# Order of the first product's units in the attention steps, and of VectorE's work where the second layer begins

## The chip, the cores and the metric

One NeuronCore of a Trainium2 chip runs the whole program: TensorE (matmuls), VectorE, ScalarE, GpSimd and SyncE (SP, which issues the loads and stores), each with its own list of instructions, bound to each other by semaphores alone. The metric is the device time of one execution in microseconds (us), from repeated runs. Beside it there is one profiled execution, whose trace gives the start and length of every instruction.

## The reference

Attention with a soft cap over 2 x 12 heads of 448 positions and 64 columns, then two feed-forward layers on the 896 tokens of width 768, with an inner width of 2048:

```python
scores = cap * tanh((q @ k.T / sqrt(64)) / cap)
attn = exp(scores - max(scores)); attn /= sum(attn) + 1e-9
x = (attn @ v) as (896, 768)
x = elu(x @ w_in) @ w_out            # first layer
x = leaky(x @ w_in2, 0.01) @ w_out2  # second layer
```

## The kernel before, in words

**Numbers in two parts.** Each f32 operand of TensorE is kept as a rounded high part (`..._hi`) and the low rest (`..._lo`), and a **product** of one 128 x 128 weight block with 448 columns is three matmuls: high x high, high weight x low data, low weight x high data (`product`, lines 1127 to 1131). The high part is made by ScalarE, the low part by a subtraction on VectorE or GpSimd, after the high part.

**Attention steps.** The attention of 24 heads is cut into 48 half heads (slots). One step `s` of 55 has, on TensorE in this order (lines 1220 to 1240): the 8 transposes of slot s-2, products of the first layer placed "before scores", the four score matmuls of slot s+1, products "before values", in odd steps 8 matmuls of values, and products "after values". ScalarE does tanh(s), the exponentials of slot s-1, `hidden(u)` for each unit that ended in step s-1, the high part of the probabilities of slot s-2, and the weight copy `w_high(u + 3)` for each such unit (lines 698 to 707). VectorE does the maxima, the end of `hidden(u)`, the low part of the probabilities (line 765) and, in turn, the reciprocals and the scaling of the outputs. From slot 23 on the transposes of a step wait for the low part of the slot before (lines 1094 to 1098). GpSimd's list has, per step (from line 568): the low part of the weights `split_w(u + 3)` of each unit that ended in the step before, in odd steps the split of v, every fourth step (the last is step 53) `x_parts(m)`, three instructions that make two parts of the attention's output, and in even steps the split of k and q.

**Units.** The first product of layer 1 (x @ w_in) is done in units, two batches of 16. Unit u is 128 of the 2048 columns; it takes KC = 6 products (u, c), c = 0 to 5, that add up in one of three PSUM banks. Product c needs the output of heads 2c and 2c+1. A unit **ends** with c = 5. Its end releases `hidden(u)` (two ScalarE instructions and one on VectorE, which free its bank), ScalarE's copy of the weights of unit u+3, GpSimd's split of the same weights (line 559), and SP's load of raw weights of unit u+7. A product waits for the split of its unit's weights. Where the products of the first batch stand is written by hand: `EARLY` (steps 24 to 30), `MIXED` (how many at each of the three places of a step) and `LATER` (in which order). Behind step 54 the 16 units of the second batch run one after the other.

**Second products, blocks.** The other three big products of the two layers use a 7-product form of the 2 x 2 block product (p1 to p7). p5, p6, p3 and p7 need sums of weight blocks (`weight_sum`, VectorE, line 880) and sums of data (`x_sum`, line 899). After the second product of layer 1 (`second(0)`), the first product of layer 2 runs in blocks i = 0 to 7 of seven, in the order `BLOCK_SEQ`: (0, p3), (0, p7), (0, p1), (0, p5), (0, p6), (1, p1), (1, p5), (1, p6), (1, p3), (1, p7), (0, p2), (0, p4), (1, p2), (1, p4), and then (2, p1) and so on; they are called items 0, 1, 2, ... Each is 3 products, 9 matmuls, into one PSUM bank; the eight banks go round, so (1, p3) takes the bank of (0, p3), and waits until `block_hidden(0, "p3")` has read it.

**The border** is the stretch in which layer 2's data are made. On VectorE `x_low(p)` (line 895) is the low part of the data of p, after ScalarE's `x_high(p)` (line 652). The data of p5, p6 and p4 are the second, third and fourth data sum. `add_to(0, "p4", ...)` (line 891) finishes the last quarter of layer 1's result. `block_add(i, p)` (lines 944 to 957) gathers the blocks' sums, ScalarE's `leak(i, p)` (line 672) scales one by 0.01, `block_hidden(i, p)` (line 962) takes the maximum and frees the bank. `block_keep(i)` (line 664) is ScalarE's copy of p1's bank, and `block_add(i, "p6")` waits for it.

ScalarE's list at the border is fixed: weight copies of items 0 and 1, `x_high("p1")`, items 2 and 3, `x_high("p5")`, items 4 and 5, `x_high("p6")`, items 6, 7, 8 and 9, `block_keep(0)`, `x_high("p2")`, items 10 and 11, `leak(0, "p3")`, item 12, `leak(0, "p7")`, item 13, `x_high("p4")`, `block_keep(1)`. A weight copy of an item with a sum waits for that sum: items 8 and 9 are (1, p3) and (1, p7). GpSimd's list is the splits of the same items.

Of the kernel before, what the change touches and what calls it, by code (L numbers as in the profile page):

```python
# [1 line left out]

# [7 lines left out]
ALU = mybir.AluOpType  # L10
# [10 lines left out]
KC = D_MODEL // P  # L21
# [3 lines left out]
MAT_UNITS = FC  # L25
# [19 lines left out]

TWO_BANKS = 10
EARLY = {24: ((0, (0, 1, 2)),), 25: ((0, (3,)),), 26: ((1, (0, 1, 2)),), 27: ((1, (3,)),), 28: ((2, (0, 1, 2)),),
         29: ((2, (3,)),), 30: ((0, (4,)), (1, (4,)), (2, (4,)))}

FIRST_LOADS = (7, 11, 15, 19, 23, 26, 29)  # L50
STEPS = 55
# [2 lines left out]

MIXED = {31: (0, 0, 1), 32: (0, 1, 0), 33: (0, 2, 0), **{s: (2, 2, 0) for s in range(34, 48, 2)},
         **{s: (1, 1, 0) for s in range(35, 48, 2)}, 48: (2, 1, 0), 49: (1, 2, 0), 50: (2, 1, 0), 51: (2, 0, 4),
         52: (0, 0, 6), 53: (0, 0, 6), 54: (0, 0, 8)}


def early_chunks(u):  # L60
# [1 line left out]

LATER = [(0, 5), (1, 5), (3, 0), (3, 1), (2, 5)] + [(u, c) for u in range(3, MAT_UNITS) for c in range(KC) if u > 3 or c > 1]


def chunks_at(s):

    if s in EARLY:  # L70
        return [], [], EARLY[s]
    done = sum(sum(n) for t, n in MIXED.items() if t < s)
    places = []
    for n in MIXED.get(s, (0, 0, 0)):
        place = {}
        for u, c in LATER[done:done + n]:
            place.setdefault(u, []).append(c)
        places.append(list(place.items()))
        done += n
    return places  # L80

# [84 lines left out]
def build(nc, qT, kT, v, w, cap, out, inv_rows):  # L166
    with ExitStack() as ctx:
# [584 lines left out]
        def _(dve):  # L752
# [89 lines left out]
            def weight_sum(n):  # L842
                stage, p, j = item_name(n)
                raws = ITEM_RAWS[n]
                for r in raws:
                    dve.wait_ge(*loaded(r))
                if stage == "blocks":
                    dst, (lo, hi) = w_source(n), (slice(0, HALF), slice(HALF, UNIT))
                    if j >= 2:
                        dve.wait_ge(*split_done(GEMM1 + BLOCK_AT[j - 2, p]))  # L850
                    else:
                        dve.wait_ge(*split_done(GEMM1 - 9))
                    if p == "p6" or p == "p3":
                        ahead = GEMM1 + BLOCK_AT[j, SUMS[SUMS.index(p) - 1]]
                        dve.wait_ge(*sum_done(ahead))
                        before = w_source(ahead)
                    a11, a12 = w_raw[:, raws[0] % RAW, lo], w_raw[:, raws[0] % RAW, hi]
                    if p == "p5":
                        args = a11, a12, ALU.add
                    elif p == "p7":  # L860
                        args = a11, w_raw[:, raws[1] % RAW, lo], ALU.subtract
                    elif p == "p6":
                        args = before, a11, ALU.subtract
                    else:
                        args = a12, before, ALU.subtract
                else:
                    dst, one = s_sum[:, j, :], w_raw[:, raws[0] % RAW, :]
                    if p == "p5":
                        if stage == "second1":
                            dve.wait_ge(*split_done(GEMM2[1] - 3))  # L870
                        args = one, w_raw[:, raws[1] % RAW, :], ALU.add
                    else:
                        dve.wait_ge(*split_done(n - PQ))
                        if p == "p7":
                            args = one, w_raw[:, raws[1] % RAW, :], ALU.subtract
                        elif p == "p6":
                            args = dst, one, ALU.subtract
                        else:
                            args = one, dst, ALU.subtract
                nc.vector.tensor_tensor(dst, *args).then_inc(s_done, 1)  # L880
# [6 lines left out]
            def add_to(l, p, dst, kept, there):  # L887

                dve.wait_ge(pair_done, product_end(l, p))
                for t in range(HC):  # L890
                    nc.vector.tensor_tensor(dst[:, t, :], kept[:, t, :], banks_of[l][p][t], ALU.add).then_inc(there, 1)

            def x_low(p):
                dve.wait_ge(xc_hi_done, X_GROUPS.index(p) + 1)
                nc.vector.tensor_tensor(x_parts_of[p][1][:, :, :], x_source[p][:, :, :], f32(x_parts_of[p][0][:, :, :]),
                                        ALU.subtract).then_inc(xc_split, 1)

            def x_sum(dst, a, b, op):
                nc.vector.tensor_tensor(dst[:, :, :], a[:, :, :], b[:, :, :], op).then_inc(x_sum_done, 1)
# [38 lines left out]
            def block_add(i, p):  # L938

                ps, u2, p1 = block_bank(i, p), block_u2[i % 2], block_p1[i % 2]  # L940
                dve.wait_ge(unit_done, product_no(i, p))
                if p == "p6":
                    dve.wait_ge(block_p1_kept, i + 1)
                    nc.vector.tensor_tensor(u2, p1, ps, ALU.add).then_inc(block_u2_done, 1)
                    dve.wait_ge(block_u2_done, i + 1)
                    nc.vector.tensor_tensor(block_u4, u2, block_bank(i, "p5"), ALU.add).then_inc(block_u4_done, 1)
                if p == "p3":
                    dve.wait_ge(block_u4_done, i + 1)
                    nc.vector.tensor_tensor(ps, block_u4, ps, ALU.add).then_inc(h_done, 1)
                if p == "p7":  # L950
                    nc.vector.tensor_tensor(u2, u2, ps, ALU.add).then_inc(block_u3_done, 1)
                    dve.wait_ge(block_u3_done, i + 1)
                    nc.vector.tensor_tensor(ps, block_u4, ps, ALU.add).then_inc(h_done, 1)
                if p == "p2":
                    nc.vector.tensor_tensor(ps, p1, ps, ALU.add).then_inc(h_done, 1)
                if p == "p4":
                    nc.vector.tensor_tensor(ps, u2, ps, ALU.add).then_inc(h_done, 1)

            def block_hidden(i, p):
                dst = {"p3": b12, "p7": b22, "p2": b11, "p4": b21}[p]  # L960
                dve.wait_ge(leak_done, quarter_no(i, p))
                nc.vector.tensor_tensor(dst[:, i, :], act_g[:, quarter_no(i, p) % 2, :], block_bank(i, p), ALU.max
                                        ).then_inc(quarter_done, 1)
# [51 lines left out]
            x_low("p1")  # L1015
            dve.wait_ge(xc_split, X_GROUPS.index("p1") + 1)
            x_sum(y12, y12, y11, ALU.subtract)
            weight_sum(GEMM1 + BLOCK_AT[1, "p3"])
            x_low("p5")
            x_sum(y11, y22, y11, ALU.add)  # L1020
            weight_sum(GEMM1 + BLOCK_AT[1, "p7"])
            x_low("p6")
            dve.wait_ge(u3_done, HC)
            add_to(0, "p4", y21, kept_u2[0], y21_done)
            for q in range(GEMM1 + 1, GEMM2[1] + 1):

                i, p = BLOCK_SEQ[q - GEMM1 - 1]
                if i == 0 and p == "p6":
                    x_low("p2")
                if p == "p6":  # L1030
                    block_add(i, "p6")
                if i == 0 and p == "p6":
                    block_add(0, "p3")
                    block_add(0, "p7")
                    block_hidden(0, "p3")
                    block_hidden(0, "p7")
                    dve.wait_ge(xc_split, X_GROUPS.index("p2") + 1)
                    x_sum(y21, y21, y11, ALU.subtract)
                if i == 1 and p == "p5":
                    x_low("p4")  # L1040
                if i and p in ("p3", "p7") or p in ("p2", "p4"):
                    block_add(i, p)
                    k = quarter_no(i, p) - 2
                    if p != "p3":
                        block_hidden(*RESULTS[k])
                if i >= 2 and p == "p1":
                    block_hidden(i - 1, "p4")

                if i == 3 and p in ("p1", "p5", "p3"):
                    c = ("p1", "p5", "p3").index(p)  # L1050
                    first_difference(1, c)
                    third_difference(1, c)
                if i >= 3 and p == "p4":
                    first_difference(1, i)
                    third_difference(1, i)
                if q + 8 < GEMM2[1] and q + 8 >= GEMM1 + 14 and q + 8 in SUM_ITEMS:
                    weight_sum(q + 8)
                if q in (GEMM2[1] - 4, GEMM2[1] - 2):
                    g_low(1, (q - GEMM2[1] + 4) // 2)
# [223 lines left out]
```

## Time and profile before

| | |
|---|---|
| median of 3 runs | 575.11 us (574.1 to 576.91) |
| profiled execution | 574.71 us, span of its trace 572.9 us |
| instructions | 8610 |
| attention steps | step 30 starts on TensorE at 99.12, step 54 at 195.23 |
| second product of layer 1 ends, blocks begin | 360.60 |
| last stall at the border ends | 383.05 |

How to read it: times in the trace are us from the start of the span. PE is TensorE, DVE VectorE, ACT ScalarE, POOL GpSimd. Matmuls overlap, so the time of one is read from start to start, not from its length. A bracket at a row's end tells how long the engine stood idle before it, and which instruction's end released it. "x4" means that four alike were merged into one row. The chain and the waits name the instruction that came last.

### The profile page before, as it was taken

Reading aid. Unit: us, or ns where it says so; the run is one execution under the profiler, and the core shown is the slowest. Engines: PE = TensorE matmul, PEld = TensorE weight load, DVE = VectorE, ACT = ScalarE, POOL = GpSimd, SP = SyncE. Lnnn points to the kernel's source line nnn. Section 1 sums busy time; section 2 is a strip of 40 time slices with the busy share of each in tenths; the row PEclk is TensorE's granted clock in tenths of the full one; section 3 lists DMA queues with packets and bytes.
Section 4 is the critical chain, followed back from the end, with each engine's and each line's share of the span. In section 5 each row is a group of like instructions: output and inputs, shape, how many; then the busy total and the mean of one; then the engine's idle time right before and its main releaser. Section 6 shows DMA issues by size and latency. Waiting matters only on the chain.

```text
span 572.9 us, 8610 instructions
## 1 busy us (share of the span) xinstructions
PE 556.7 (97%) x2908; PEld 499.4 (87%) x2908; DVE 469.4 (82%) x758; ACT 352.8 (62%) x606; POOL 275.2 (48%) x273
## 2 busy tenths in 40 slices
PE   6999989999999999999999999989999999999997
PEld 5777779889998999999999999879999998999997
DVE  5899998878875133898988999889999779999881
ACT  6999988999995455654644454536454445544440
POOL 6779998799965655552000003856666530000000
DMA  6455564455423333335644332031113225536251
GB/s 174 106 143 128 150 174 125 123 130 146 98 65 89 98 112 110 111 108 165 213 135 158 131 99 67 1 110 56 57 55 90 77 84 192 159 119 220 84 170 51
DMA packets 34172, 67.07 MB, mean 117 GB/s; under 512 B 6864, under 2 KB 18768, under 8 KB 34128
## 3 DMA queue, kind: packets, MB, share of 16 engines
q1 hardware_dynamic: 33984, 66.28, 39.4%
q8 instruction: 24, 0.39, 0.3%
q14 instruction: 20, 0.16, 0.1%
q10 hardware_dynamic: 144, 0.23, 0.1%
HBM read 63.70 MB, written 2.80 MB: 116 GB/s over the span
## 4 chain that ended last, share of the span: by engine, by line
PE 77%; DVE 10%; ACT 4%; issue 3%; POOL 3%; DMA 2%; ACTq 0%; SPq 0%; DVEq 0%; POOLq 0%
PE mlp_ps L1129 8%; PE mlp_ps L1131 8%; PE mlp_ps L1130 8%; PE o_ps L1129 6%; PE o_ps L1131 6%; PE o_ps L1130 6%; PE scores L1129 4%; PE scores L1130 4%; PE scores L1131 4%; PE probs_t L1103 4%; PE probs_t L1131 4%; PE probs_t L1130 4%; PE probs_t L1129 4%; PE scores L1088 2%; PE o_ps L1122 2%
## 5 line engine op out<-in xcount | busy, mean ns | idle before, releaser
L559 POOL TENSOR_TENSOR w_lo<-w_raw,w_hi 128x768 fp32r<-128x768 f32 (+1 forms) x62 | 104.2, 1681 | 62.3 <-ACT w_hi L621 61.9
L559 POOL TENSOR_TENSOR w_lo<-s_sum,w_hi 128x384 fp32r<-128x384 f32 x32 | 38.8, 1228 | 114.5 <-ACT w_hi L621 114.5
L621 ACT ACTIVATE w_hi<-s_sum 128x768 fp32r<-128x768 f32 (+1 forms) x64 | 43.4, 684 | 76.6 <-DVE s_sum L880 51.9
L621 ACT ACTIVATE w_hi<-w_raw 128x768 fp32r<-128x768 f32 (+1 forms) x77 | 56.5, 737 | 31.1 <-PE o_ps L1131 15.7
L601 ACT ACTIVATE soft<-soft,neg_max 112x448 f32<-112x448 f32 x96 | 63.6, 673 | 1.8 <-DVE soft L758 1.7
L758 DVE TENSOR_SCALAR_CACHE_REDUCE soft<-soft,neg_abs 112x448 f32<-112x448 f32 x96 | 60.9, 671 | 2.2 <-ACT soft L591 1.9
L1129 PE MATMUL mlp_ps<-x_hi,w_hi 128*128 128x448 f32 x132 | 49.2, 373 | 0.4 <-issue 0.4
L765 DVE TENSOR_TENSOR p_lo<-probs_t,p_hi 112x896 fp32r<-112x896 f32 x37 | 40.3, 1089 | 10.0 <-ACT p_hi L610 9.9
L1130 PE MATMUL mlp_ps<-x_lo,w_hi 128*128 128x448 f32 x132 | 48.2, 365 | 0.0
L1131 PE MATMUL mlp_ps<-x_hi,w_lo 128*128 128x448 f32 x132 | 48.2, 365 | 0.0
L591 ACT ACTIVATE soft<-scores 112x896 f32<-112x896 f32 x47 | 43.4, 924 | 6.0 <-PE scores L1089 5.9
L1088 PE MATMUL scores<-k_hi,q_stack 128*112 128x448 f32 x94 | 36.7, 390 | 4.6 <-ACT soft L591 2.8
L1103 PEld LDWEIGHTS probs_t<-ident,soft 112*112 112x112 f32 x296 | 30.5, 133 | 8.5 <-issue 4.1
L1103 PE MATMUL probs_t<-ident,soft 112*112 112x112 f32 x296 | 34.6, 260 | 3.0 <-DVE p_lo L765 2.3
L610 ACT ACTIVATE p_hi<-probs_t 112x896 fp32r<-112x896 f32 x37 | 33.9, 916 | 5.5 <-PE probs_t L1103 5.5
L803 DVE SCALAR_TENSOR_TENSOR b<-act_g,mlp_ps 128x448 f32<-128x448 f32 x22 | 13.6, 619 | 28.6 <-ACT act_g L630 28.5
L1089 PE MATMUL scores<-k_lo,q_stack 128*112 128x448 f32 x94 | 34.3, 365 | 0.0
L880 DVE TENSOR_TENSOR s_sum<-w_raw 128x768 f32<-128x768 f32 (+1 forms) x32 | 29.4, 920 | 3.8 <-DMA w_raw<-w_units 2.1
L884 DVE TENSOR_TENSOR w_lo<-s_sum,w_hi 128x768 fp32r<-128x768 f32 x32 | 30.4, 950 | 1.5 <-ACT w_hi L621 1.5
L839 DVE TENSOR_TENSOR g_first<-b,g_first 128x896 fp32r<-128x896 f32 x24 | 29.9, 1247 | 0.8 <-ACT g_first L640 0.8
L839 DVE TENSOR_TENSOR g_last<-b,g_last 128x896 fp32r<-128x896 f32 x24 | 27.8, 1160 | 2.2 <-ACT g_last L640 2.2
L628 ACT ACTIVATE act_g<-mlp_ps 128x448 f32<-128x448 f32 x22 | 11.9, 540 | 24.9 <-PE mlp_ps L1131 24.9
(238 smaller groups left out, 1747.7 us busy)
## 6 DMA issues: line engine op xcount, KB each, us to landing
w_raw<-w_units SPq DMA_DIRECT2D x120, 384.0 KB, 3.2
q_raw<-qT SPq DMA_DIRECT2D x24, 224.0 KB, 3.1
k_raw<-kT SPq DMA_DIRECT2D x23, 224.0 KB, 3.0
v_raw<-v_rows SPq DMA_DIRECT2D x24, 112.0 KB, 3.2
inv_all<-inv_rows SPq DMA_DIRECT2D x24, 112.0 KB, 3.4
y_t<-y_out SPq DMA_DIRECT2D x12, 224.0 KB, 2.8
inv_rows<-row_inv SPq DMA_DIRECT2D x24, 1.8 KB, 3.1
k_raw<-kT ACTq DMA_DIRECT2D x1, 224.0 KB, 3.1
```

The source lines that it names most:

```text
L559: pool.tensor_tensor(w_part(w_lo, n), w_source(n), f32(w_part(w_hi, n)), ALU.subtract).then_inc(w_lo_pool, 1)
L591: nc.scalar.activation(soft[0:QT, k % SOFT, :, :], scores_of(k)[0:QT, :, 0:SEQ], ACT.Tanh, scale=scale_reg).then_inc(tanh_done, 1)
L601: nc.scalar.activation(soft[0:QT, b, t, :], soft[0:QT, b, t, :], ACT.Exp, bias=neg_max[:, c, t:t + 1], scale=-1.0, accum_out=row_sum[:, h ...
L621: nc.scalar.activation(w_part(w_hi, n), w_source(n), ACT.Copy).then_inc(w_hi_done, 1)
L758: nc.vector.tensor_scalar(soft[0:QT, b, t, :], soft[0:QT, b, t, :], neg_abs[0:QT, 0:1], BIG, ALU.mult, ALU.min, accum_out=neg_max[:, c, t: ...
L765: nc.vector.tensor_tensor(p_lo[:, h % 2, :, cols].rearrange("p (a b) q -> p a b q", a=2), probs_of(k)[0:QT, :, 0:SEQ].rearrange("p a (b q) ...
L839: nc.vector.tensor_tensor(parts[:, 2:4, :], g_source(l, n)[0], f32(parts[:, 0:2, :]), ALU.subtract).then_inc(g_split, 1)
L1088: nc.tensor.matmul(dst[0:QT, t, 0:SEQ], q_stack[:, b, rows], k_hi[:, b, :], start=True, stop=False)
L1103: last = nc.tensor.transpose(probs_of(k)[0:QT, c // 2, col:col + 2 * QT - 1:2], soft[0:QT, k % SOFT, t, c * QT:(c + 1) * QT], ident[:, :])
L1129: nc.tensor.matmul(dst, w_hi[:, r, blk], hi, start=start, stop=False)
L1130: nc.tensor.matmul(dst, w_hi[:, r, blk], lo, start=False, stop=False)
L1131: return nc.tensor.matmul(dst, w_lo[:, r, blk], hi, start=False, stop=stop)
```

## The change

Three things change, and nothing is added or taken away in what is computed.

First, the order of the first batch's products. Before, a unit's last product (c = 5) came ahead of the first product of the next unit but one, and units 0 to 3 ended in steps 31, 32, 34 and 35. Now c = 4 and 5 of a unit come among the first products of the next: unit u ends in step 2u + 31 up to unit 9 (31, 33, 35, ... 49), units 10, 11 and 12 in steps 51, 52 and 53, and 13, 14 and 15 in step 54 (before: unit 3 in 35, 4 in 37, ... 10 in 49, 11 in 51, 12 in 52, 13 in 53, 14 and 15 in 54). Step 30 has one product in place of three, step 54 ten in place of eight. Step 54 is now (14, 3), (13, 5), (14, 4), (15, 0 to 3), (14, 5), (15, 4), (15, 5). `chunks_at` groups only neighbours of the same unit, so that this order is kept.

Second, on VectorE, ahead of the blocks: the third data sum directly behind the second; `weight_sum` of (1, p7) behind the three adds of p4.

Third, on VectorE, in block 0: `x_low("p2")` behind the adds of p6 and p3 instead of ahead of them, and `block_hidden(0, "p3")` ahead of `block_add(0, "p7")`.

```diff
-         29: ((2, (3,)),), 30: ((0, (4,)), (1, (4,)), (2, (4,)))}
+         29: ((2, (3,)),), 30: ((0, (4,)),)}
...
-         52: (0, 0, 6), 53: (0, 0, 6), 54: (0, 0, 8)}
+         52: (0, 0, 6), 53: (0, 0, 6), 54: (0, 0, 10)}
...
-LATER = [(0, 5), (1, 5), (3, 0), (3, 1), (2, 5)] + [(u, c) for u in range(3, MAT_UNITS) for c in range(KC) if u > 3 or c > 1]
+LATER = [(0, 5), (1, 4), (1, 5), (3, 0), (2, 4), (3, 1), (3, 2), (3, 3), (2, 5), (3, 4)] + [
+    chunk for u in range(4, MAT_UNITS) for chunk in [(u, c) for c in range(4)] + [(u - 1, 5), (u, 4)]] + [(MAT_UNITS - 1, 5)]
...
-        place = {}
-        for u, c in LATER[done:done + n]:
-            place.setdefault(u, []).append(c)
-        places.append(list(place.items()))
+        runs = itertools.groupby(LATER[done:done + n], lambda chunk: chunk[0])
+        places.append([(u, [c for _, c in run]) for u, run in runs])
...
             x_sum(y12, y12, y11, ALU.subtract)
+            x_sum(y11, y22, y11, ALU.add)
             weight_sum(GEMM1 + BLOCK_AT[1, "p3"])
             x_low("p5")
-            x_sum(y11, y22, y11, ALU.add)
-            weight_sum(GEMM1 + BLOCK_AT[1, "p7"])
             x_low("p6")
             dve.wait_ge(u3_done, HC)
             add_to(0, "p4", y21, kept_u2[0], y21_done)
+            weight_sum(GEMM1 + BLOCK_AT[1, "p7"])
             for q in range(GEMM1 + 1, GEMM2[1] + 1):
...
-                if i == 0 and p == "p6":
-                    x_low("p2")
                 if p == "p6":
                     block_add(i, "p6")
                 if i == 0 and p == "p6":
                     block_add(0, "p3")
+                    x_low("p2")
+                    block_hidden(0, "p3")
                     block_add(0, "p7")
-                    block_hidden(0, "p3")
                     block_hidden(0, "p7")
```

## Rows read from the trace of the kernel before

**Rows 1.** the page, part 1: busy us (share of the span) xinstructions, of TensorE.
```profile
PE 556.7 (97%) x2908; PEld 499.4 (87%) x2908; DVE 469.4 (82%) x758; ACT 352.8 (62%) x606; POOL 275.2 (48%) x273
```

**Rows 2.** windows by attention step, TensorE: us, busy us (xmatmuls), clock, DMA.
```profile
99.12:102.52 3.40, 3.40 (x23) 1.00 0.08 23
...
106.34:109.78 3.44, 2.35 (x17) 1.00 0.24 67
109.78:114.46 4.68, 4.59 (x27) 1.00 0.40 124
...
118.50:122.93 4.43, 4.43 (x28) 1.00 0.43 125
122.93:127.51 4.58, 4.20 (x26) 1.00 0.60 117
...
131.95:135.97 4.02, 4.02 (x26) 1.00 0.43 121
```

**Rows 3.** timeline, border, TensorE: start us, us, engine line op tiles [idle <-releaser].
```profile
368.28 0.44 PE L1129 MATMUL scores<-p_hi,w_hi 128*128 128x448 f32 x1 [0.22 <-DVE p_lo L895]
...
377.03 0.47 PE L1129 MATMUL o_ps<-p_hi,w_hi 128*128 128x448 f32 x1 [1.22 <-DVE b L962]
...
383.05 0.44 PE L1129 MATMUL scores<-p_hi,w_hi 128*128 128x448 f32 x1 [0.28 <-DVE p_lo L895]
```

**Rows 4.** timeline, steps 53 and 54, TensorE: the first matmul of two products.
```profile
192.80 0.36 PE L1129 MATMUL o_ps<-x_hi,w_hi 128*128 128x448 f32 x1
...
195.23 0.36 PE L1129 MATMUL o_ps<-x_hi,w_hi 128*128 128x448 f32 x1
```

**Rows 5.** timeline, steps 30 and 32, VectorE: the low part of the probabilities.
```profile
101.04 1.09 DVE L765 TENSOR_TENSOR p_lo<-probs_t,p_hi 112x896 fp32r<-112x896 f32 x1 [0.93 <-ACT p_hi L610]
...
108.54 1.09 DVE L765 TENSOR_TENSOR p_lo<-probs_t,p_hi 112x896 fp32r<-112x896 f32 x1 [0.19 <-ACT p_hi L610]
```

**Rows 6.** timeline, steps 53 and 54, GpSimd: x_parts(11) begins, and the split behind it.
```profile
193.13 1.17 POOL L549 TENSOR_TENSOR x_raw<-x_raw,inv_all 128x448 f32<-128x448 f32 x1
...
196.15 1.84 POOL L559 TENSOR_TENSOR w_lo<-w_raw,w_hi 128x768 fp32r<-128x768 f32 x1
```

**Rows 7.** timeline, border, VectorE.
```profile
359.85 1.37 DVE L880 TENSOR_TENSOR s_sum<-w_raw,s_sum 128x384 f32<-128x384 f32 x1
...
362.80 2.38 DVE L899 TENSOR_TENSOR y<-y 128x1344 f32<-128x1344 f32 x1
...
366.57 1.56 DVE L895 TENSOR_TENSOR p_lo<-y,p_hi 128x1344 fp32r<-128x1344 f32 x1
...
371.12 2.23 DVE L895 TENSOR_TENSOR p_lo<-u_first,p_hi 128x1344 fp32r<-128x1344 f32 x1 [1.39 <-ACT p_hi L652]
373.27 0.61 DVE L944 TENSOR_TENSOR u_even<-p_even,scores 128x448 f32<-128x448 f32 x1
...
374.64 0.63 DVE L949 TENSOR_TENSOR o_ps<-block_u,o_ps 128x448 f32<-128x448 f32 x1
...
376.36 1.32 DVE L962 TENSOR_TENSOR b<-act_g,o_ps 128x448 f32<-128x448 f32 x2
377.60 2.35 DVE L899 TENSOR_TENSOR u_first<-u_first,y 128x1344 f32<-128x1344 f32 x1
```

**Rows 8.** timeline, border, GpSimd: weight splits.
```profile
358.48 2.33 POOL L559 TENSOR_TENSOR w_lo<-s_sum,w_hi 128x384 fp32r<-128x384 f32 x1
...
363.72 2.34 POOL L559 TENSOR_TENSOR w_lo<-w_raw,w_hi 128x384 fp32r<-128x384 f32 x1
367.03 4.90 POOL L559 TENSOR_TENSOR w_lo<-s_sum,w_hi 128x384 fp32r<-128x384 f32 x4 [0.97 <-ACT w_hi L621]
```

**Rows 9.** timeline, border, ScalarE: four weight copies, block_keep(0), one leak.
```profile
366.44 1.75 ACT L621 ACTIVATE w_hi<-s_sum 128x384 fp32r<-128x384 f32 x4
368.10 0.52 ACT L664 ACTIVATE p_even<-mlp_ps 128x448 f32<-128x448 f32 x1
...
376.49 0.54 ACT L672 ACTIVATE act_g<-o_ps 128x448 f32<-128x448 f32 x1 [0.23 <-DVE o_ps L953]
```

More of the change, by code:

```diff
@@ L1 @@
 from contextlib import ExitStack
+import itertools
 import numpy as np
```

## The prediction

> **What bounds it now.** I read first the busy shares of the page: TensorE is busy 556.7 us of the span [rows 1], and its clock is 1.00 in every stretch read, so time can come only from the few places where it stands still, or from making new ones. Then the windows of the attention steps, TensorE alone [rows 2]: a step is as long as its work (3.40, 4.43, 4.02) except three: 3.44 where the same work is two products shorter than in 3.40, 4.68 beside 4.43, 4.58 beside 4.02. The stalls are 1.26 (3.44 less 3.40 - 1.22), 0.25 and 0.56 us, at the ends of steps 32, 33 and 36. Then the timeline at the border to the blocks: TensorE waits there three times for VectorE [rows 3]. With the restart after each wait (a start against its place in an even row of products) that is about 0.38, 1.37 and 0.43 us. Both parts of the change aim at these six places, together some 4.2 us.
>
> **Step stage: what moves.** No work is added or removed. A product is three matmuls, 0.61 us (four of them between the two starts of [rows 4]). Steps 24 to 29 stay. Step 30 loses two products, step 54 gains two (+1.22 us there), all others keep their number. From step 32 on each unit ends one or two steps later, and its ScalarE pair, VectorE result, weight split on GpSimd and load on SP move with it.
>
> Step 30: its work falls to 3.40 - 1.22 = 2.18. The next transposes need the low part of this step's probabilities: that starts at 101.04 [rows 5], and in the row where TensorE waited for it the transposes follow 109.78 - 108.54 = 1.24 later [rows 2, 5]. So step 31 can start at 102.28 instead of 102.52: only 0.24 of the 1.22 is won, a new stall of 0.98 us. Step 31 is then bound by TensorE; step 32 has one product in both kernels and unit 0 still ends in step 31, so its stall of 1.26 stays. Steps 33 to 36: before, units 0 to 3 ended in steps 31, 32, 34, 35 and ScalarE had four units in five steps; a unit every second step leaves it room, and I let both later stalls go: -0.25 and -0.56. At step 37 the new kernel is 0.24 + 0.25 + 0.56 = 1.05 ahead of the old clock. Steps 38 to 53 have the same shape, with u one lower. The weight slack shrinks from about four steps to three, which at some 4.2 us a step still covers the 1.8 us split. SP's waits for free raw buffers shift by whole units and its attention loads stay in place.
>
> Step 54 is where I see harm. GpSimd runs, in this order, a weight split, x_parts(11) from 193.13, and the next split from 196.15 to 197.99 [rows 6]. These stand for units 15 and 16 before, and for 14 and 15 after, since every unit ends one place later and releases the same position in GpSimd's queue. Product (15, 0) is now the fourth of step 54; on the old clock that step starts at 195.23 [rows 4] and the product is wanted at 195.23 + 3 x 0.61 = 197.06. Its weights are there at 197.99, TensorE goes on about 0.06 later: a stall of 0.99. (Unit 14 just passes: its first product is wanted 0.61 after 192.80, at 193.41, and its split ends by 193.17.) Unit 16's split comes before the ten products are through.
> Sum of the stage: -1.05 + 1.22 + 0.99 = **+1.16 us**. Bounds: -0.8 if both new stalls find cover, +2.0 if the two old ones stay as well.
>
> **Border: what moves.** Two lists are touched. On VectorE the third data sum (y11, source of p6) goes ahead of the weight sum of (1, p3) and x_low(p5); the weight sum of (1, p7) goes behind the three adds of p4; x_low(p2) goes behind the first three adds of block 0, and block_hidden(0, p3) ahead of block_add(0, p7). Nothing moves on ScalarE, GpSimd or SP, but they wait on what moved.
>
> The rows show how VectorE and GpSimd share: from 358.48 to 366.1 they take turns. A GpSimd split needs 0.97 (four of them from 368.05, where x_low ends, to 371.93) but takes 2.33 or 2.34, a data sum needs 1.47 (365.18 less 363.72) but takes 2.38, a weight sum needs 0.43 and takes 1.37 [rows 7, 8]: each waits for the other's whole instruction, and a waiting GpSimd gets its turn between two VectorE instructions that follow at once. The page "SBUF — State Buffer" of the Trainium skill (Who interferes with whom) says that a VectorE instruction with two SBUF inputs and a GpSimd instruction that reads SBUF block each other fully, and that issue order decides. It does not say who goes first when both are waiting; if VectorE kept its turn, the border would come out near the first rival below. The rows have GpSimd next, so my sum alternates. Instructions with a PSUM input (0.61) are not stretched.
>
> By these turns the new order runs: data sum y11 issued 359.85, GpSimd's split ends 358.48 + 2.33 = 360.81, sum done 362.28. ScalarE can now round p6 from 362.3 (before 365.2, since the sum ended at 365.18). Split until 363.25, weight sum (1, p3) until 363.68, split until 364.65, x_low(p5) until 366.12, split until 367.1, x_low(p6) until 368.6. Before, the next instruction followed its start by 1.48, at 368.05: the old order met GpSimd idle twice, waiting for ScalarE, and the new one has taken that idleness away. One turn more (0.97) and one sum fewer (0.43) is +0.54. TensorE starts 1.71 after the undisturbed start of an x_low (366.57 to 368.28 [rows 3, 7]): (0, p5) at 366.38, 0.3 late, (0, p6) at 368.82.
>
> Then three adds until 370.2, and the weight sum (1, p7), behind one more split, until about 371.0. ScalarE's list has the weight copy of (1, p7) as the last of a run of four, **ahead of** block_keep(0) and x_high(p2). Before, all four ran from 366.44 and block_keep stood at 368.1 [rows 9]; now ScalarE is held until 371.0, block_keep(0) comes at 371.4 and x_high(p2) from 371.9 to 373.2. block_add(0, p6) needs block_keep: it starts at 372.0 (before 373.27), and by the old spacing (374.64 + 0.63 - 373.27 = 2.0) the sum for p3 is ready at 374.0. x_low(p2) meets the split of item 10, whose weight copy follows x_high(p2) at once; GpSimd is about 0.2 ahead, so x_low(p2) ends at 376.15 instead of 375.4. block_hidden(0, p3) starts there and releases (1, p3) 377.03 - 376.36 = 0.67 later, at 376.8: 0.2 better than before [rows 3, 7]. Then two adds (1.27), leak on ScalarE (0.54 [rows 9], which nothing covers any more), block_hidden(0, p7) 378.65 to 379.27, so (1, p7) waits once more, 0.6. The fourth data sum is issued at 379.25 instead of 377.60. From that issue to product (0, p4) it was 383.05 - 377.60 = 5.45 with a turn of 0.88 lost to GpSimd; now it is about the same (the split of item 13 starts at 379.1), so (0, p4) starts at 384.67.
> Sum of the border: 384.67 - 383.05 = **+1.62 us**. Bounds: -2.2 if all three stalls go, +2.5 if each of the two later links loses another turn (0.97).
>
> Behind (0, p4) both engines' chains shift together and I see no slack that takes it back; SP's next loads wait for the splits of items 10 and 11, which come up to 2 us later, still ahead of the first sum of block 2.
>
> **The sum.** +1.16 + 1.62 = +2.8 us on the profiled 574.71, which is 0.4 under the median; on the median of 575.11 it gives 577.9. A measurement of this kernel tells about 0.5% (2.9 us) from no change, so the forecast is slower, at the very edge of what can be seen.
>
> **Rivals.**
> - Both parts do what they are built for. Price: -0.8 and -2.2, 572.1. It needs GpSimd to leave VectorE the next turn: then x_low(p6) is done near 365, ScalarE is released near 367 instead of 371.0, and block 0's adds wait only for TensorE. For it: VectorE idled 1.39 before x_low(p2) [rows 7], which vanishes. Against it: the turns in [rows 7, 8]. 0.11. It decides at x_low(p5): if that instruction takes 1.56 and not 2.4, this case holds.
> - The step stage costs as summed, the border gains part (0 to -2.2), for instance because the split of item 10 comes behind x_low(p2) and GpSimd idles elsewhere: 574.1 to 576.3. 0.17.
> - The step stage is harmless (-0.8) because the latency of (15, 0) is hidden, the border as summed: 575.9. 0.13.
> - Worse: ScalarE's wait for the weight sum also delays the splits that free block 0's raw rows, SP loads block 2 late, and its sums stand in TensorE's way. It decides if the first of those rows lands after 384.5, when VectorE comes to its first sum; price about +2 more, 580. 0.13.
> - The forecast itself, within 1.2 either way: 0.46. About four parts in seven of it lie inside 0.5%.
>
> **Numbers.** Faster by over 0.5%: part of the first rival, 0.07. Slower by over 0.5%: the fourth and part of the forecast, 0.35. Within: 0.58. The range leaves out most of the first rival below and the tail above 580.2: 574.1, the low end of the second rival, to 580.2.
>
> **What would show it.** In the changed profile: TensorE idle about 1 us ahead of the transposes of step 31 and none after step 33; idle about 1 us ahead of the first product of unit 15, with GpSimd's split as releaser; ScalarE idle some 5 us for the weight sum of (1, p7) ahead of block_keep(0); x_low(p5) stretched to about 2.4 us; (0, p4) later against the end of the second product by about 1.6. The prediction is wrong if (0, p6) starts without a stall, or if unit 15 finds its weights.

## The result, and the profile after

The changed kernel takes 576.51 us (median of 20 runs, 574.96 to 578.49), the kernel before 574.50 (20 runs, 573.35 to 576.91). The ratio is 1.0035, 95% interval 1.0025 to 1.0045: about 2.0 us slower. The prediction said 577.9 on a base of 575.11, that is +2.8 us, slower at the edge of what can be seen. The difference is clear of the noise, and inside the 0.5% that the prediction took for the limit. The profiled execution took 577.36 us, span 575.6, against 574.71 and 572.9. Of these 2.65 us, 0.67 lie ahead of step 30, where both kernels do the same (its transposes start at 99.79, before at 99.12 [rows 2]), and are no part of the change. All fourteen profiles of this document run the same program up to step 30, and it starts anywhere from 98.59 to 102.11. The granted clock of the first 14 us is 0.90 in this profile and 1.00 in the one before; it is 0.91 in the profile of short_splits too, whose step 30 comes at 98.59, so the clock alone doesn't set the start.

The page of the changed kernel, busy times, against [rows 1]:

```profile
PE 559.4 (97%) x2908; PEld 501.6 (87%) x2908; DVE 470.4 (82%) x758; ACT 353.4 (61%) x606; POOL 275.9 (48%) x273
```

The same instructions, and waits in other places. Line numbers on the engines ahead of TensorE are one higher than before (an import was added). The timeline of TensorE in the changed kernel, the start of steps 30, 31 and 33, then unit 15's and unit 16's first product:

```profile
99.79 0.93 PE L1103 MATMUL probs_t<-ident,soft 112*112 112x112 f32 x8
...
102.95 0.95 PE L1103 MATMUL probs_t<-ident,soft 112*112 112x112 f32 x8 [0.81 <-DVE p_lo L766]
...
110.24 0.95 PE L1103 MATMUL probs_t<-ident,soft 112*112 112x112 f32 x8 [1.09 <-DVE p_lo L766]
...
197.68 0.47 PE L1129 MATMUL mlp_ps<-x_hi,w_hi 128*128 128x448 f32 x1 [0.80 <-POOL w_lo L560]
...
202.04 0.36 PE L1129 MATMUL mlp_ps<-x_hi,w_hi 128*128 128x448 f32 x1
```

The first product of unit 16 before, and the windows of steps 33 and 36 in the changed kernel (us, busy us, matmuls, granted clock, DMA), against 4.68 and 4.58 in [rows 2]:

```profile
200.09 0.36 PE L1129 MATMUL mlp_ps<-x_hi,w_hi 128*128 128x448 f32 x1
```

```profile
110.24:114.69 4.45, 4.45 (x27) 1.00 0.52 143
123.15:127.18 4.03, 4.03 (x26) 1.00 0.50 127
```

Step 30 lasts 3.16 in place of 3.40, and behind its work TensorE waits for the low part of the probabilities; the wait ahead of step 33 is the old one; those ahead of steps 34 and 37, at the ends of these two windows, have gone. At 197.68 it waits for GpSimd. From the start of step 30 to unit 16 it is 102.25, before 100.97 (99.12 to 200.09): **+1.28 us** from the steps. GpSimd in the same stretch of the changed kernel: the split of unit 14, x_parts(11), and only then the split of unit 15:

```profile
190.98 1.85 POOL L560 TENSOR_TENSOR w_lo<-w_raw,w_hi 128x768 fp32r<-128x768 f32 x1 [3.42 <-ACT w_hi L622]
192.78 1.17 POOL L550 TENSOR_TENSOR x_raw<-x_raw,inv_all 128x448 f32<-128x448 f32 x1
...
195.80 1.82 POOL L560 TENSOR_TENSOR w_lo<-w_raw,w_hi 128x768 fp32r<-128x768 f32 x1
```

At the border, TensorE of the changed kernel: the first product of the blocks, and then the four that waited, (0, p6), (1, p3), (1, p7) and (0, p4), against [rows 3]:

```profile
362.55 0.37 PE L1129 MATMUL o_ps<-p_hi,w_hi 128*128 128x448 f32 x1
...
370.21 0.44 PE L1129 MATMUL scores<-p_hi,w_hi 128*128 128x448 f32 x1 [0.20 <-DVE p_lo L896]
...
378.03 0.47 PE L1129 MATMUL o_ps<-p_hi,w_hi 128*128 128x448 f32 x1 [0.28 <-DVE b L963]
...
380.46 0.47 PE L1129 MATMUL o_ps<-p_hi,w_hi 128*128 128x448 f32 x1 [0.33 <-DVE b L963]
...
385.76 0.44 PE L1129 MATMUL scores<-p_hi,w_hi 128*128 128x448 f32 x1 [1.39 <-DVE p_lo L896]
```

The blocks begin at 362.55 (before 360.60). From there to (0, p4) it is 23.21, before 22.45: **+0.76 us**. The wait of (1, p3) shrank from 1.22 to 0.28 and two others took its place. VectorE and ScalarE there, against [rows 7] and [rows 9]:

```profile
359.63 4.56 DVE L900 TENSOR_TENSOR y<-y 128x1344 f32<-128x1344 f32 x2
364.11 1.37 DVE L881 TENSOR_TENSOR s_sum<-w_raw,s_sum 128x384 f32<-128x384 f32 x1
365.40 4.67 DVE L896 TENSOR_TENSOR p_lo<-y,p_hi 128x1344 fp32r<-128x1344 f32 x2
369.99 0.61 DVE L892 TENSOR_TENSOR u_first<-u_first,probs_t 128x448 f32<-128x448 f32 x1
...
371.58 0.74 DVE L881 TENSOR_TENSOR s_sum<-w_raw 128x384 f32<-128x384 f32 x1
373.42 0.62 DVE L945 TENSOR_TENSOR u_even<-p_even,scores 128x448 f32<-128x448 f32 x1 [1.09 <-ACT p_even L665]
...
379.78 0.62 DVE L963 TENSOR_TENSOR b<-act_g,o_ps 128x448 f32<-128x448 f32 x1 [0.61 <-ACT act_g L673]
380.32 2.34 DVE L900 TENSOR_TENSOR u_first<-u_first,y 128x1344 f32<-128x1344 f32 x1
```

```profile
372.36 0.53 ACT L622 ACTIVATE w_hi<-s_sum 128x384 fp32r<-128x384 f32 x1 [5.57 <-DVE s_sum L881]
372.79 0.53 ACT L665 ACTIVATE p_even<-mlp_ps 128x448 f32<-128x448 f32 x1
```

To be read in this: both x_lows now take a turn of GpSimd each (4.67 for the two, 1.56 each before). ScalarE stands 5.57 us for the weight sum of (1, p7), its next instruction is block_keep(0), and VectorE's block_add(0, p6) waits 1.09 for that. Further down VectorE waits 0.61 for the leak, and the fourth data sum is issued 17.77 after the blocks begin (380.32), before 17.00.

+1.28 and +0.76 are 2.04 us. The medians say 2.0, with an interval of 1.4 to 2.6. Behind (0, p4) nothing is lost or won in these two profiles: to the start of the last matmul it is 186.49 us before and 186.43 after. That one profile of each kernel meets the medians so closely is in part luck, since profiles of one kernel differ by more than this change (last section).

### The profile page after: what moved, and what is told of

It reads as the page before. It is cut to its first block, busy times and chain, and to the rows that moved or that the text cites. A ratio compares the mean times of both kernels' runs of the same rounds, so it can differ in the third digit from the quotient of the medians.

```text
span 575.6 us, 8619 instructions
## 1 busy us (share of the span) xinstructions
PE 559.4 (97%) x2908; PEld 501.6 (87%) x2908; DVE 470.4 (82%) x758; ACT 353.4 (61%) x606; POOL 275.9 (48%) x273
## 4 chain that ended last, share of the span: by engine, by line
PE 73%; DVE 12%; ACT 7%; issue 4%; DMA 2%; POOL 1%; DVEq 0%; ACTq 0%; POOLq 0%
PE mlp_ps L1129 8%; PE mlp_ps L1130 8%; PE mlp_ps L1131 8%; PE o_ps L1129 6%; PE o_ps L1131 6%; PE o_ps L1130 6%; PE scores L1129 4%; PE scores L1131 4%; PE scores L1130 4%; PE probs_t L1103 4%; PE probs_t L1129 4%; PE probs_t L1131 4%; PE probs_t L1130 4%; ACT soft L602 3%; DVE p_lo L896 2%
## 5 line engine op out<-in xcount | busy, mean ns | idle before, releaser
L1129 PEld LDWEIGHTS mlp_ps<-x_hi,w_hi 128*128 128x128 f32 x132 | 24.8, 188 | 3.9 <-POOL w_lo L560 1.2
```

What stands on the lines that cost most here:

```text
L1129: nc.tensor.matmul(dst, w_hi[:, r, blk], hi, start=start, stop=False)
```

## The experiments

Eight kernels were timed, and four profiles repeat three of the kernels. All ratios are to the kernel before. Beside the ratio stands what the trace fixes more sharply: the time from the first product of the blocks to (0, p4), 22.45 before and 23.21 after, called the border below. steps_only, border_only, late_parts and sum_back were timed in one series, in which the kernel before took 575.84 us; the other four in a second, in which it took 575.92. Times in us are compared within a series, ratios across.

**The parts alone.** steps_only has the new order of units and the old border; border_only has the old steps and the new border.

> Only the first part of the change: the new order of the units in the attention steps, the border as in the kernel before. My account of the two traces: the blocks begin 1.95 us later in the changed kernel, of which 0.67 was there before step 30 began (not from the change), so this part costs 1.3 us. Expected: +1.3 us against the kernel before (ratio 1.0022). Rival A (nearly all of the loss is the border's, the step stage only looks longer because its profiled run began late): ratio 1.000. Rival B (all of the loss is the step stage's and the border's shift is compensated later): +2.0 us, ratio 1.0035. In the trace: TensorE idle 0.8 us ahead of step 31 and ahead of unit 15's first product, none at the ends of steps 33 and 36.

Measured 1.0037 (1.0023 to 1.0051), 577.89 us. 

> Only the second and third part: VectorE's order at the border and in block 0, the attention steps as before. Expected from the traces: product (0, p4) starts 0.76 us later against the start of the blocks, and nothing takes it back: +0.8 us (ratio 1.0013). Rival A (the whole loss is here): +2.0 us, ratio 1.0035. Rival B: 0. steps_only and this should add up to the changed kernel's +2.0.

Measured 1.0005 (0.9992 to 1.0018), 576.20 us; border 23.18. The waits of steps_only are as expected (0.80 ahead of step 31, 0.81 ahead of unit 15), and in border_only the border's shift is the changed kernel's. That the whole loss is the border's (rival A of both) is ruled out, and so is a step stage without cost. Rival B of both is not ruled out by the times: the interval of steps_only holds 1.0035 and leaves the expected 1.0022 just outside, and that of border_only holds 1.0000 as well as 1.0013. That the border costs its part rests on the traces alone: 23.18 in place of 22.45, and from (0, p4) to the start of the last matmul 186.46, before 186.49, so nothing takes it back. A likely reason for the high time of steps_only is told with the repeated profiles.

**GpSimd's queue ahead of unit 15.** late_parts:

```diff
 def x_step(m):
+    if m == PAIRS - 1:
+        return STEPS - 1
     return 4 * m + (9 if 2 * m >= DIRECT else 11)
```

> The changed kernel, but GpSimd does x_parts(11) one step later, behind the weight split of unit 15 instead of ahead of it. If GpSimd's queue is what unit 15's first product waits for, the 0.97 us stall goes: 1.0 us faster than the changed kernel, so +1.0 against the kernel before (ratio 1.0018). The split of unit 16 now stands behind x_parts(11) and ends about when unit 16 wants it, which could give back up to 0.3. Rival (the stall is due to the weight copy on ScalarE or the load): no gain, ratio 1.0035.

Measured 1.0029 (1.0015 to 1.0043), 577.45 us. GpSimd's timeline, then the first product of unit 16:

```profile
193.87 1.85 POOL L562 TENSOR_TENSOR w_lo<-w_raw,w_hi 128x768 fp32r<-128x768 f32 x1 [1.80 <-ACT w_hi L624]
195.68 1.18 POOL L552 TENSOR_TENSOR x_raw<-x_raw,inv_all 128x448 f32<-128x448 f32 x1
...
198.70 1.84 POOL L562 TENSOR_TENSOR w_lo<-w_raw,w_hi 128x768 fp32r<-128x768 f32 x1
```

```profile
200.59 0.48 PE L1131 MATMUL mlp_ps<-x_hi,w_hi 128*128 128x448 f32 x1 [0.22 <-POOL w_lo L562]
```

Unit 15 no longer waits, unit 16 now does, 0.39 us. From the start of step 31 to unit 16 it is 98.37 (102.22 to 200.59), in the changed kernel 99.09, before 97.57. So the queue is what unit 15 waited for, and 0.72 comes back: the stall of 0.97 and the 0.1 of its restart, less the new one of 0.39. The timing alone could not have shown it, its interval takes in both expectations.

**What holds ScalarE.** sum_back:

```diff
+            weight_sum(GEMM1 + BLOCK_AT[1, "p7"])
             dve.wait_ge(u3_done, HC)
             add_to(0, "p4", y21, kept_u2[0], y21_done)
-            weight_sum(GEMM1 + BLOCK_AT[1, "p7"])
```

> The changed kernel with the weight sum of (1, p7) ahead of the three adds of p4 again (behind x_low(p6)); the third data sum stays early. My theory: ScalarE is held by that sum ahead of block_keep(0) and x_high(p2). The sum then ends 1.5 us earlier, block_add(0, p6) can start when (0, p6) and the adds are done, about 1.0 us earlier, and so does everything down to (0, p4): 0.9 us faster than the changed kernel, ratio 1.0019; ScalarE's wait for the sum falls from 5.6 us to about 4. Rival (the turns with GpSimd and x_low(p2)'s new place make the loss, not the wait): no gain, or 0.3 slower because the adds come 0.7 later, ratio 1.0035 to 1.004.

Measured 1.0014 (1.0000 to 1.0028), 576.22 us; border 22.05, that is 1.16 less than in the changed kernel. ScalarE, and what TensorE then waited for, ahead of (0, p6), (1, p1) and (0, p4):

```profile
373.19 0.53 ACT L622 ACTIVATE w_hi<-s_sum 128x384 fp32r<-128x384 f32 x1 [4.58 <-DVE s_sum L881]
373.62 0.53 ACT L665 ACTIVATE p_even<-mlp_ps 128x448 f32<-128x448 f32 x1
```

```profile
372.02 0.44 PE L1129 MATMUL scores<-p_hi,w_hi 128*128 128x448 f32 x1 [0.16 <-DVE p_lo L896]
374.80 0.47 PE L1129 MATMUL probs_t<-p_hi,w_hi 128*128 128x448 f32 x1 [0.70 <-DVE u_first L892]
386.45 0.44 PE L1129 MATMUL scores<-p_hi,w_hi 128*128 128x448 f32 x1 [0.44 <-DVE p_lo L896]
```

The place of one 0.4 us sum was worth more than the whole loss of the border: with it put back, the border is 0.4 shorter than before, although the adds now come late (0.70 ahead of (1, p1)). The rival falls; the interval of the ratio holds the expected 1.0019 and ends below the rival's 1.0035.

**The turns of VectorE and GpSimd.** short_splits leaves out the low parts of columns 128 to 383 of items 3 to 13:

```diff
+                cols = slice(0, HALF // 3 if GEMM1 + 3 <= n < GEMM1 + 14 else None)
-                pool.tensor_tensor(w_part(w_lo, n), w_source(n), f32(w_part(w_hi, n)), ALU.subtract).then_inc(w_lo_pool, 1)
+                pool.tensor_tensor(w_part(w_lo, n)[:, cols], w_source(n)[:, cols], f32(w_part(w_hi, n))[:, cols], ALU.subtract
+                                   ).then_inc(w_lo_pool, 1)
```

> The changed kernel, but GpSimd splits only the first 128 of the 384 columns of items 3 to 13, so each of its turns is about 0.35 us in place of 0.97; the low parts of the other columns are left out. My theory (each instruction of VectorE with two SBUF inputs waits out one whole turn of GpSimd): the instructions that now take 2.3 take about 1.8, (0, p6) starts without a stall, ScalarE gets the sum of (1, p7) over 1.5 us sooner, and (0, p4) starts 2.6 us sooner than in the changed kernel, about 20.6 after the blocks begin: ratio 0.999. Rival (VectorE's own work and ScalarE's order bind, the turns hardly matter): (0, p4) at 23.2 as in the changed kernel, ratio 1.0035.

Measured 0.9976 (0.9952 to 0.9999), 573.69 us; border 20.56. VectorE's two data sums, the weight sum and the two x_lows, and ScalarE's wait:

```profile
358.38 3.99 DVE L902 TENSOR_TENSOR y<-y 128x1344 f32<-128x1344 f32 x2
362.30 0.55 DVE L883 TENSOR_TENSOR s_sum<-w_raw,s_sum 128x384 f32<-128x384 f32 x1
362.77 3.55 DVE L898 TENSOR_TENSOR p_lo<-y,p_hi 128x1344 fp32r<-128x1344 f32 x2
```

```profile
368.42 0.52 ACT L624 ACTIVATE w_hi<-s_sum 128x384 fp32r<-128x384 f32 x1 [3.13 <-DVE s_sum L883]
```

Nothing on VectorE was changed, and its two x_lows fell from 4.67 to 3.55, the weight sum from 1.37 to 0.55. From start to start an x_low with a turn takes 1.74, in the changed kernel 2.30. The border came out at 20.56 for an expected 20.6, although the turns were 0.42 and not the expected 0.35, so that it hit so well is in part luck. GpSimd's turns set the length of VectorE's instructions here.

**Block 0's order.** block0_only is the third part of the change on the kernel before; sum_first goes one step on:

```diff
                     block_hidden(0, "p3")
                     block_add(0, "p7")
+                    dve.wait_ge(xc_split, X_GROUPS.index("p2") + 1)
+                    x_sum(y21, y21, y11, ALU.subtract)
                     block_hidden(0, "p7")
-                    dve.wait_ge(xc_split, X_GROUPS.index("p2") + 1)
-                    x_sum(y21, y21, y11, ALU.subtract)
```

> The kernel before with only the third part of the change: x_low(p2) behind the adds of p6 and p3, and block_hidden(0, p3) ahead of block_add(0, p7). Expected: block 0's sums come sooner and the 1.37 us stall ahead of (1, p3) goes, but the fourth data sum still stands at the end of the same list of VectorE, so (0, p4) starts within 0.3 us of its old place, 22.45 us after the blocks begin, and its own stall grows from 0.43 to about 1.8: no change in time, ratio 1.000. Rival (this part is what makes the changed border 0.76 slower): (0, p4) at 23.2, ratio 1.0013.

Measured 0.9989 (0.9971 to 1.0007), 575.09 us; border 22.04. 

> As block0_only, and the fourth data sum between block_add(0, p7) and block_hidden(0, p7), where VectorE otherwise idles until ScalarE's leak is done. If the end of the border hangs on when the fourth data sum is issued, (0, p4) starts about 0.9 us sooner than before, near 21.5 after the blocks begin, at the price of about 0.9 us of stall ahead of (1, p7): ratio 0.9985. Rival (TensorE is bound by the banks freed by block_hidden, not by the data sum): no gain, ratio 1.000 or more.

Measured **0.9968 (0.9953 to 0.9983)**, 573.88 us; border 21.32. TensorE's waits, first block0_only, (0, p6) and (0, p4), then sum_first, (0, p6) and (1, p7):

```profile
368.12 0.44 PE L1128 MATMUL scores<-p_hi,w_hi 128*128 128x448 f32 x1 [0.20 <-DVE p_lo L895]
382.51 0.44 PE L1128 MATMUL scores<-p_hi,w_hi 128*128 128x448 f32 x1 [1.13 <-DVE p_lo L895]
```

```profile
368.84 0.44 PE L1128 MATMUL scores<-p_hi,w_hi 128*128 128x448 f32 x1 [0.21 <-DVE p_lo L895]
378.74 0.47 PE L1128 MATMUL o_ps<-p_hi,w_hi 128*128 128x448 f32 x1 [0.36 <-DVE b L962]
```

The third part by itself takes the wait of (1, p3) away, and nearly all of it turns up ahead of (0, p4): the border is 0.4 shorter (0.3 at most was expected), not the 1.37 of the stall. What sets the end is when the fourth data sum is issued: from there to (0, p4) it is 5.44 or 5.45 us in all nine profiles in which (0, p4) waits and GpSimd's splits are whole (two of the changed kernel, the kernel before, steps_only twice, border_only, late_parts, sum_back, block0_only), whatever came ahead. Put into the gap in which VectorE waits for the leak, it takes 1.13 us off the border of the kernel before, 0.72 more than block0_only, and (0, p4) waits no longer. This kernel beats both; 1.13 us of its 1.8 are placed by the trace, and its interval (1.0 to 2.7 us) holds them.

**A version for the steps too.** nine_early adds late_parts and this order to sum_first:

```diff
-         29: ((2, (3,)),), 30: ((0, (4,)), (1, (4,)), (2, (4,)))}
+         29: ((2, (3,)),), 30: ((0, (4,)), (1, (4,)))}
...
+LATER = [(0, 5), (2, 4), (1, 5), (3, 0), (3, 1), (3, 2), (3, 3), (3, 4), (2, 5), (4, 0)] + [
+    chunk for u in range(4, MAT_UNITS - 1) for chunk in [(u, 1), (u, 2), (u, 3)]
+    + ([(u, 4), (u - 1, 5)] if u < 11 else [(u - 1, 5), (u, 4)]) + [(u + 1, 0)]] + [
+    (MAT_UNITS - 1, 1), (MAT_UNITS - 2, 5)] + [(MAT_UNITS - 1, c) for c in range(2, 6)]
```

> A version meant to beat both: the border of sum_first, x_parts(11) one step later, and an order of units in which one ends in every second step while step 30 keeps two products (step 54 has nine). Expected in the steps: the stalls at the ends of steps 33 and 36 (0.25 and 0.56) go, step 31 starts 0.24 sooner, 0.61 us of work goes to step 54, unit 15 doesn't wait, unit 16 waits up to 0.4: between -0.4 and 0.0 us. With the border's -0.9: -1.3 to -0.9 us against the kernel before, ratio 0.998. Rival (a new stall at step 35 or in steps 52 to 54 takes the gain): ratio 1.000 or more.

Measured 0.9991 (0.9967 to 1.0015), 575.86 us, with runs from 571.88 to 578.50. From step 31 to unit 16 it is 97.82, 0.25 more than before, and step 31 comes 0.24 sooner: nothing won in the steps, the upper end of what was expected, because unit 16 waits 0.37. The border is that of sum_first in both repeated profiles below (21.32 and 21.31), so the traces place 1.1 us of gain, ratio 0.998; the interval holds this as well as the rival's 1.000, and the median shows no gain. None of it explains a spread of 6.6 us.

**Repeated profiles.** In the profiles of steps_only and nine_early TensorE was slower from unit 16 to the border, 160 us in which it never waits. Four more were taken.

> The same kernel as nine_early, for one more profile. In nine_early the pace of TensorE (start to start of the three matmuls of a product) was 0.620 us from the 0.36 us stall ahead of unit 16 up to the border (202 to 364), in the kernel before 0.608 there. Theory: the pace is drawn anew at each restart of TensorE after a stall and then holds through the dense stage, so the same kernel shows either. Expected: 0.608 or 0.620 from 202 on, constant up to the border; with 0.608 the blocks begin about 3 us sooner after unit 16's start. Rival (the pace belongs to the program): 0.620 again in every profile of it.

> A third profile of the same kernel, as nine_again_a: theory, either pace; rival, 0.620.

> The changed kernel once more, for a second profile. Its first one ran at 0.608 from unit 15's stall (197) to the border. Theory: may show 0.620 there this time, and then its border has smaller stalls, since VectorE is less behind TensorE; the structural distances (0.97 ahead of step 31, 0.97 ahead of unit 15) repeat within 0.02. Rival: 0.608 again.

> steps_only once more: its first profile ran at 0.620 from unit 15's stall to the border and its span was 579.6, which is where its ratio of 1.0037 in place of the expected 1.0022 may come from. Theory: 0.608 or 0.620; with 0.608 the blocks begin about 3 us sooner after the stall. Rival: 0.620 again.

Windows of TensorE (us, busy us, matmuls, granted clock, DMA): first steps_only, then the same kernel as steps_again.

```profile
205.00:225.00 20.00, 20.00 (x98) 1.00 0.36 103
245.00:265.00 20.00, 20.00 (x99) 1.00 0.33 98
...
400.00:420.00 20.00, 20.00 (x99) 1.00 0.26 79
```

```profile
205.00:225.00 20.00, 20.00 (x100) 1.00 0.36 104
245.00:265.00 20.00, 20.00 (x101) 1.00 0.38 108
...
400.00:420.00 20.00, 20.00 (x101) 1.00 0.19 59
```

From the restart at unit 15 to the border, three matmuls took 0.620 us in steps_only and 0.608 in steps_again, at a granted clock of 1.00 in both. In nine_early it was 0.620 from its restart at unit 16, in nine_again_a and nine_again_b 0.608. The pace is not the program's; that rival falls. (That it is drawn only at a restart is not borne out either: see the last section.) Of the 4.0 us between the spans of steps_only and steps_again (579.6 and 575.6), 3.2 lie between unit 16 and the border. nine_early and its repeats have spans of 574.4, 573.0 and 570.4. after_again showed 0.608 up to the border like the first profile, and its distances repeat: 0.98 ahead of step 31, 0.98 ahead of unit 15, border 23.18. Yet its span is 578.2, against 575.6: 1.3 us lie ahead of step 30, and 1.3 behind (0, p4), where it had the slow pace from 497 to the end and the first profile didn't.

## Why the prediction was right, point by point

- **Step 31 bound by the low part of the probabilities**: forecast a start 0.24 sooner and a stall of 0.98; measured 0.24 and 0.97.
- **The stall ahead of step 33 stays, the two later ones go**: measured 1.24, none and none. Forecast 1.05 ahead at step 37; measured 1.0 there and still at step 49 (176.23 less the 0.67, against 176.57).
- **Unit 15 waits for GpSimd's split behind x_parts(11)**: forecast 0.99, measured 0.97, with GpSimd as releaser; late_parts shows the queue to be the cause.
- **Sum of the steps**: forecast 1.16, measured 1.28. The lead was 0.04 smaller, and the matmul behind the stall of unit 15 is followed after 0.31 in place of 0.20, a restart that the sum had left out.
- **At the border the third sum comes sooner, but (0, p6) doesn't**: forecast 0.54 later against the blocks' begin; measured 7.66 (362.55 to 370.21), before 7.68. (0, p5), forecast 0.3 late, is not late at all. Here the sum failed in size: a term of +0.54 was nothing.
- **ScalarE held by the sum of (1, p7), block_keep(0) late**: forecast an idle time of some 5 us, measured 5.57; sum_back shows the price.
- **(1, p7) waits once more for the leak, the fourth data sum is issued late, (0, p4) with it**: all three are there; 0.50 for a forecast 0.6, and +0.76 for a forecast +1.62.

The term that was mis-sized is the turn of GpSimd: "Split until 363.25, weight sum (1, p3) until 363.68, split until 364.65, x_low(p5) until 366.12". I added the whole times that each engine's instruction takes alone, 0.97 and 1.47 or 0.43. The starts in the trace say 364.11, 365.40 and 369.99: a weight sum with a turn costs 1.29, an x_low with a turn 2.30, where I had 1.40 and 2.44. For the long instructions the old trace would have given it, read from start to start (362.80 to the next instruction at 365.10 is 2.30); for the weight sums it would not, they stand 1.47 apart from the next start there (365.10 to 366.57). Over the instructions up to x_low(p6) that makes 0.56 of the 0.86 us: four turns of GpSimd in 8.18 us, where the old order took 8.19 with three and one weight sum more. The rest is in the later links: block_hidden(0, p3) follows 2.03 behind the start of x_low(p2), where I had 2.15, and the fourth data sum 2.95 behind block_hidden(0, p3), where I had 3.10.

The first rival, in which VectorE keeps the turn, asked for an x_low(p5) of 1.56; the pair took 4.67. The page "SBUF — State Buffer" of the Trainium skill (Who interferes with whom) leaves open who is next when both wait; in every turn read here it was the engine that had waited. That the loser is blocked for the whole instruction, as the page has it, agrees with short_splits but for some 0.15 us: from start to start an x_low loses 0.83 us to a split of 0.97, and there 0.26 to a split of 0.42.

The rival that block 2's loads come late did not happen: behind (0, p4) the time to the last matmul is the old one (186.43 and 186.49).

## What to carry to other kernels

Before an instruction is moved back on one engine, read the other engine's fixed list: what waits for it holds everything behind itself, wanted or not, and here a 0.4 us sum moved by three adds cost over 1 us through ScalarE's order. A stall that is removed is gained only up to the next thing that was late anyway; find what sets the end of the stretch (here the issue of the fourth data sum), and move that. When two engines block each other by turns, take the price from start to start, and expect that an engine which is released sooner will take more turns. Before a difference of less than 0.5% is put down to a change, compare the pace of TensorE in the same stretch of both profiles.

## What the runs showed of the hardware that was not expected

TensorE has two paces for the same 128 x 448 matmuls at a granted clock of 1.00: 0.608 or 0.620 us for three, 2% apart. It is not fixed by the program: steps_only and nine_early each showed both in the same stretch. In the windows read from 205 to the border the pace held from beginning to end, and in steps_only it changed exactly with the restart at unit 15's stall. A wait is not needed for a change, though: in nine_again_b it went to 0.620 near 192.4, between two products, and back to 0.608 with the restart at unit 16. From unit 16 to the border (160 us) the slow pace costs about 3 us, more than all that this change did.

The later stretches show it too, and in the kernel before as well. From the restart at (0, p4) to the next restart some 90 us later, five of the fourteen profiles ran at 0.620 (before, both of the changed kernel, steps_only, sum_back); from about 500 to the end again five (after_again, block0_only, border_only, nine_again_a, sum_first). Windows of TensorE, first the kernel before and block0_only, then the changed kernel and after_again:

```profile
400.00:440.00 40.00, 40.00 (x196) 1.00 0.20 60
400.00:440.00 40.00, 40.00 (x199) 1.00 0.20 60
...
500.00:540.00 40.00, 40.00 (x199) 1.00 0.49 154
500.00:540.00 40.00, 40.00 (x195) 1.00 0.47 149
```

The load of the DMA engines is nearly the same in each pair (0.20 and 0.20, 0.49 and 0.47), so this load doesn't explain the pace. The first profiles of the kernel before and of the changed one happen to have the slow pace in the same stretch and nowhere else behind unit 16, which is why they could be compared link by link. An estimate from these stretches: all three slow instead of fast, some 330 us at 2%, is over 6 us, about the spread of nine_early's runs.

In the four profiles without a wait near unit 15 or 16 (before, border_only, block0_only, sum_first) the stretch from there to the border ran at 0.608; of the ten with one, two ran at 0.620. So a short wait ahead of a long dense stretch may cost more than its length, and this may be why steps_only came out at 1.0037 for distances that place 1.0022. But two of ten against none of four can as well be chance, and the later stretches are slow in kernels of every kind. That is argued, not shown, and what picks the pace stays open.
